# Pausing a fused attention and two-layer MoE kernel twice per block instead of four times

## What is computed

```python
# attention over chunks of 32 queries, 4 batches, 8 heads, 768 tokens, head size 64
k_full = concat(mem_k, k[l_start:r_end])          # 8 memory keys + up to 56 near keys
a = softmax(scale * q_c @ k_full.T);  out = a @ v_full
x = out as (3072, 512)
# first MLP
h = x @ w_in                                      # (3072, 2048)
g = h * sigmoid(h);  y = g @ w_out                # (3072, 512)
# soft MoE: 32 slots, 8 experts
logits = y @ phi                                  # (3072, 32)
d = softmax(logits, over tokens);  slot_input = d.T @ y
slot_out[e] = relu(slot_input[e] @ w1[e]) @ w2[e]
result = softmax(logits, over slots) @ slot_out
```

## Time and profile before

| | us |
|---|---|
| median of 3 executions | 465.17 (465.12 to 467.6) |
| profiled execution | 469.86 |
| span of the profiled execution | 467.9 |
| PE busy in that span | 448.6 |
| DVE busy | 276.7 |
| ACT busy | 138.9 |

### The profile page before, as it was taken

The page is one execution under the profiler, slowest core; times in us unless marked ns, Lnnn a source line. Parts: engine busy times, 40 slices in busy tenths (PEclk is TensorE's granted clock), DMA queues, the critical chain, the costliest instruction groups (busy, mean ns, idle before and its releaser), DMA issues.

```text
span 467.9 us, 12260 instructions
## 1 busy us (share of the span) xinstructions
PE 448.6 (96%) x5438; PEld 332.6 (71%) x5438; DVE 276.7 (59%) x540; ACT 138.9 (30%) x257; POOL 47.4 (10%) x44
## 2 busy tenths in 40 slices
PE   6799999999999999999999999999999999999990
PEld 5699777777876787767777777787677878543560
DVE  4567558765596566766665785568644557541142
ACT  2475233232331322332332323323222222210031
POOL 2576000000000000000000000000000000010000
PEclk9899999999999999999999999999999999999997
DMA  8996232321142143303321132130160479999997
GB/s 293 411 415 276 101 117 88 104 91 54 59 193 72 37 188 102 103 2 102 104 97 49 59 102 61 46 133 1 30 242 0 182 284 424 395 420 422 420 399 295
DMA packets 14820, 81.59 MB, mean 174 GB/s; under 512 B 1584, under 2 KB 1712, under 8 KB 8880
## 3 DMA queue, kind: packets, MB, share of 16 engines
q1 hardware_dynamic: 14768, 80.81, 45.0%
HBM read 74.51 MB, written 6.29 MB: 173 GB/s over the span
## 4 chain that ended last, share of the span: by engine, by line
PE 92%; DMA 3%; DVE 2%; issue 1%; ACT 0%; DVEq 0%
PE h_ps L310 57%; PE o_ps L294 5%; PE lpu_ps L327 5%; PE sx_ps L269 4%; PE lpu_ps L360 4%; DMA qk_sb<-qk 3%; PE sx_ps L360 2%; PE pt_ps L280 2%; PE sx_ps L699 2%; PE h_ps L1013 2%; PE lpu_ps L699 2%; PE h_ps L734 1%; PE h_ps L951 1%; PE o_ps L993 1%; PE lpu_ps L370 1%; PE pt_ps L1013 1%
## 5 line engine op out<-in xcount | busy, mean ns | idle before, releaser
L310 PE MATMUL h_ps<-x_odd,w_pair 128*128 128x512 f32 x576 | 138.3, 394 | 0.0
L310 PEld LDWEIGHTS h_ps<-x_odd,w_pair 128*128 128x128 f32 x576 | 106.3, 188 | 27.8 <-issue 4.6
L545 DVE SCALAR_TENSOR_TENSOR gT<-gT,h_ps 128x512 f32<-128x512 f32 (+1 forms) x108 | 66.1, 612 | 93.1 <-ACT gT L427 93.0
L427 ACT ACTIVATE gT<-h_ps 128x512 f32<-128x512 f32 (+1 forms) x108 | 58.4, 541 | 178.1 <-PE h_ps L310 177.4
L310 PE MATMUL h_ps<-x_even,w_pair 128*128 128x512 f32 x384 | 92.5, 395 | 0.0
L310 PEld LDWEIGHTS h_ps<-x_even,w_pair 128*128 128x128 f32 x384 | 70.9, 188 | 16.8 <-issue 1.7
L555 DVE STREAM_TRANSPOSE gB<-gT 128x512 f32<-128x512 f32 x80 | 56.7, 709 | 1.8
L310 PE MATMUL h_ps<-x_short,w_pair 128*128 128x256 f32 x384 | 51.6, 288 | 1.0 <-DVE gT L545 0.5
L310 PEld LDWEIGHTS h_ps<-x_short,w_pair 128*128 128x128 f32 x384 | 47.7, 192 | 6.0 <-issue 3.6
L529 POOL TENSOR_TENSOR sc<-sc,row_stats 128x512 f32<-128x512 f32 x23 | 24.0, 1044 | 275.0 <-DVE row_stats L523 275.0
L447 ACT ACTIVATE sc<-sc 128x512 f32<-128x512 f32 x23 | 14.6, 633 | 53.2 <-DVE sc L512 49.1
(11 more groups left out here) (193 smaller groups left out, 383.6 us busy)
## 6 DMA issues: line engine op xcount, KB each, us to landing
unit<-w SPq DMA_DIRECT2D x31, 1024.0 KB, 9.6
qk_sb<-qk SPq DMA_DIRECT2D x24, 640.0 KB, 5.4
v_sb<-v SPq DMA_DIRECT2D x24, 512.0 KB, 3.6
out<-unit SPq DMA_DIRECT2D x6, 1024.0 KB, 7.2
w_stage<-w_in SPq DMA_DIRECT2D x4, 1024.0 KB, 12.0
wot<-w_outT SPq DMA_DIRECT2D x4, 1024.0 KB, 12.7
unit<-w_out SPq DMA_DIRECT2D x4, 1024.0 KB, 5.3
unit_acc<-w SPq DMA_DIRECT2D x1, 1024.0 KB, 8.7
```

The costliest lines, as they stand in the source:

```text
L310: last = nc.tensor.matmul(h_ps[k % 2][:, 0:TOKS[b]], w_pair[:, k // 2, w, kc, k % 2 * 128:k % 2 * 128 + 128], x[:, lo, kc, 0:TOKS[b]], sta ...
L427: nc.scalar.activation(gt_of(b, k), h_ps[k % 2][:, 0:TOKS[b]], ACT.Tanh, scale=0.5).then_inc(tanh_done, 1)
L545: nc.vector.scalar_tensor_tensor(out=gt_of(b, k), in0=gt_of(b, k), scalar=1.0, in1=h_ps[k % 2][:, 0:TOKS[b]], op0=ALU.add, op1=ALU.mult).t ...
```

## The change

Long blocks pause twice, after chunks 1 and 9. A pause is values of two units, two logits steps (eight chunks of g) and scores of two units. The transposes of the pair stand apart: after chunks 7 and 8, and after chunk 15 and chunk 0 of the next block. The dispatch stays after chunk 4, now without transposes beside it. For this

- the ring of g has ten chunks; it takes the memory of the two early places, so no late weights are loaded in the middle any more. The list of places still has 23 entries of its own;
- scores of the two units of a pair lie beside each other in the same PSUM banks (`s_col`); DVE reads them only when both are written. Even units' values go to `o_ps`, odd units' to `pt_ps`; probabilities and `pt` have two buffers;
- block 0 keeps its pauses but scores units 3; 4; 5 and 6; 7 there, so that unit 6 follows unit 5 at once and units 6 and 7 are ready as a pair for block 1. Two logits steps follow its chunk 15 instead of three, behind the transposes of unit 6;
- SP loads both units' `qk` and then both units' `v`.

```diff
-GT_RING = 6
+GT_RING = 10
+LAST_RING = 12
+def pair_at(b, n):
+    if b >= LAST or 2 * n >= UNITS[b + 1]:
+        return ()
+    return (FIRST[b + 1] + 2 * n, FIRST[b + 1] + 2 * n + 1)
+def scored_at(b, n):
+    if b == 0:
+        return ((3,), (4,), (5, 6), (7,))[n]
+    return pair_at(b, 1) if n == 0 else pair_at(b + 1, 0)
...
+        def s_col(u):
+            return 4 * WIN * (u % 2) if u >= 2 else 0
...
         def pe_scores(pe, u, dispatched=0):
             pe.wait_ge(qk_in[u % QK_RING], 16 * (u // QK_RING + 1))
             if u >= 2:
-                pe.wait_ge(sc_done, u)
+                pe.wait_ge(sc_done, u - 1 if u >= PAIRED and u % 2 else u)
...
+        def pe_first_block(pe):
+            for k in range(NCH):
+                pe_mlp(pe, 0, k)
+                n = k // 4
+                if k % 4 == 1:
+                    pe_probs_T(pe, first_values(n))
+                if k % 4 == 2:
+                    for u in scored_at(0, n):
+                        pe_scores(pe, u)
+                    pe_values(pe, first_values(n))
+                if k == 11:
+                    pe_w2(pe)
+                if k == 12:
+                    pe_w2_T(pe)
+                if k == 15:
+                    pe_probs_T(pe, PAIRED)
+                    for m in range(2):
+                        pe_logits(pe, 0, m)
         def pe_block(pe, b):
             for k in range(NCH):
                 pe_mlp(pe, b, k)
...
+                n = k // 8
+                if k in (0, 8) and pair_at(b, n):
+                    pe_probs_T(pe, pair_at(b, n)[1])
+                if k == 2:
+                    pe_fold(pe, b - 1)
+                if k == DISPATCH_STEP:
+                    pe_dispatch(pe, b - 1, FIRST[b + 1] + 4 if b < LAST - 1 else NUN)
+                if k in (1, 9):
+                    for u in pair_at(b, n):
+                        pe_values(pe, u)
+                    if k == 1:
+                        pe_logits(pe, b - 1, 2)
+                        pe_logits(pe, b - 1, 3)
+                    elif b < LAST:
+                        pe_logits(pe, b, 0)
+                        pe_logits(pe, b, 1)
+                    for u in scored_at(b, n):
+                        pe_scores(pe, u, b if k > DISPATCH_STEP else 0)
+                if b == LAST and k in (5, 9, 13):
+                    pe_logits(pe, b, k // 4 - 1)
+                if k == 7 and pair_at(b, 1):
+                    pe_probs_T(pe, pair_at(b, 1)[0])
+                if k == 15 and pair_at(b + 1, 0):
+                    pe_probs_T(pe, pair_at(b + 1, 0)[0])
...
         def dve_scores(dve, u):
-            dve.wait_ge(s_mm, u + 1)
+            dve.wait_ge(s_mm, u + 2 if u >= PAIRED + 2 and u % 2 == 0 else u + 1)
...
-            nc.vector.memset(pt[:], 0.0).then_inc(pt_zero, 1)
+            nc.vector.memset(pt_all[:], 0.0).then_inc(pt_zero, 1)
...
-        EARLY = 2
-        places = [(13, p_tr, 2), (12, w2t_mm, 1), (6, h_mm, NCH * (LAST - 1))] + [(i, o_mm, NUN) for i in range(3)]
-        places += [(3, h_mm, NCH * LAST), (4, h_mm, NCH * LAST)]
-        for m in range(NCH // 2):
-            places.append((14 + m, h_mm, NCH * LAST + 2 * (m + 1)))
-            if m == 1:
-                places += [(i, u_mm, NB - 1) for i in (9, 10, 11)]
-        places += [(5, h_mm, NCH * NB), (7, u_mm, NB), (8, u_mm, NB), (22, uf_mm, 1)]
+        places = [(7, h_mm, NCH * (LAST - 1))] + [(i, o_mm, NUN) for i in range(4)]
+        places += [(4, h_mm, NCH * LAST), (5, h_mm, NCH * LAST), (13, h_mm, NCH * LAST + 2), (21, parthi_done, LAST)]
+        places += [(14, h_mm, NCH * LAST + 4)] + [(i, u_mm, NB - 1) for i in (10, 11, 12)]
+        places += [(13 + m, h_mm, NCH * LAST + 2 * (m + 1)) for m in range(2, NCH // 2)]
+        places += [(6, h_mm, NCH * NB), (8, u_mm, NB), (9, u_mm, NB), (22, uf_mm, 1)]
...
-            for u in range(7, NUN):
+            load_qk(7)
+            load_v(7)
+            for u in range(8, NUN, 2):
                 load_qk(u)
+                load_qk(u + 1)
                 load_v(u)
-                if u in (12, 14):
-                    load_unit((u - 12) // 2)
-            for u in range(EARLY, len(places)):
+                load_v(u + 1)
+            for u in range(len(places)):
                 load_unit(u)
```

More of the change, by code:

```diff
@@ L145, in moe_program @@
-        stage = at("w_stage", R + 14 * HALF_W, [128, NCH // 2, 2, KC, 256])
-        units = [at(f"unit{i}", R + i * HALF_W, [128, HALF_W]) for i in range(22)]
+        sc_all = at("sc", R, [128, SB, 2 * PAIRS, WIN])
+        pt_all = at("pt", R + 1024, [128, SB, 4 * PAIRS, QT])
+        qk_sb = at("qk_sb", R + 3072, [128, QK_RING, 2, QKW])
+        v_sb = at("v_sb", R + 3072 + QK_RING * 2 * QKW, [128, V_RING, 2, H * D])
+        assert 3072 + QK_RING * 2 * QKW + V_RING * 2 * H * D <= 4 * HALF_W
@@ L147, in moe_program @@
+        stage = at("w_stage", R + 13 * HALF_W, [128, NCH // 2, 2, KC, 256])
+        units = [at(f"unit{i}", R + i * HALF_W, [128, HALF_W]) for i in range(21)]
+        units.append(at("unit_gT", 4800 + 6 * TMAX, [128, HALF_W]))
         units.append(at("unit_acc", 1536, [128, HALF_W]))
-        fold_r = at("fold_r", R + 22 * HALF_W, [128, 128], fp32r)
-        w2_last = at("w2_last", R + 22 * HALF_W + 128, [128, 128])
+        wot = [units[i] for i in (10, 11, 12, 7)]
+        fold_r = at("fold_r", R + 21 * HALF_W, [128, 128], fp32r)
@@ L344, in pe_fold @@
             if b == LAST - 1:
[L345 removed]
+                pe.wait_ge(x_done, NUN)
             pe.wait_ge(fold_rounded, 1)
@@ L613, in dve_w2_T, with dve_first_block @@
             nc.vector.tensor_copy(w2c[:], heads(lp_ps[:])).then_inc(w2_done, 1)
+        def dve_first_block(dve):
+            for k in range(NCH):
+                n = k // 4
+                if k % 4 == 3:
+                    dve_sums(dve, scored_at(0, n)[0])
+                if k == 12:
+                    dve_sums(dve, PAIRED)
+                dve_g(dve, 0, k)
+                if k % 4 == 2:
+                    dve_scores(dve, scored_at(0, n)[0])
+                    dve_x(dve, first_values(n))
+                if k == 10:
+                    dve_scores(dve, PAIRED)
+                if k == 11:
+                    dve_w2(dve)
+                if k == 12:
+                    dve_w2_T(dve)
+                dve_gb(dve, 0, k)
         def dve_block(dve, b):
             for k in range(NCH):
-                n, at_pause = k // 4, k % 4 == pause(b)
-                if k % 4 == pause(b) + 1 and scores_at(b, n) is not None:
-                    dve_sums(dve, scores_at(b, n))
-                if b and k == 3:
+                n = k // 8
+                pair, scored = pair_at(b, n), scored_at(b, n)
+                if k in (2, 10) and scored:
+                    dve_scores(dve, scored[1])
+                if k == 3:
                     dve_et(dve, b - 1)
-                if 0 < b < LAST and k == 3:
+                if k == 3 and b < LAST:
                     dve_raw(dve, b - 1, range(4))
@@ L841, in _ @@
             act_wh(act, 2)
-            for b in range(NB):
+            act_first_block(act)
+            for b in range(1, NB):
                 act_block(act, b)
@@ L883, in _ @@
             dve_sums(dve, 2)
-            for b in range(NB):
+            dve_first_block(dve)
+            for b in range(1, NB):
                 dve_block(dve, b)
@@ L965, in _ @@
             keep_busy(4, h_ps[0])
-            for b in range(NB):
+            pe_first_block(pe)
+            for b in range(1, NB):
                 pe_block(pe, b)
```

182 lines of the change are left out of this document (87 added, 95 removed).

## The result

The changed kernel takes 470.25 us (median of 4, 468.57 to 473.37) against 465.7 for the kernel before: ratio 1.0102, 95% interval 1.0074 to 1.013. It is 1% slower, where 461.4 and faster was forecast.

A forecast was written before the change was run, and what follows sets the result against it. PE was taken to bound the middle and DMA the end. Gains of 1.40 + 1.44 + 0.64 + 2.20 - 0.20 = 5.5 us, less a 1.7 halt, took 465.17 to 461.4 us; range 459.5 to 464.8.

The forecast's parts named there:

- The middle's gain: From about 40 to 367 us, where PE never waits: merged pauses gain 5.5 us; a long block takes some 61.7.
- Logits joins: Long blocks' logits steps in pairs: each join saves 0.14 us, 10 pairs, 1.4 us.
- the values': Values of two units in a row: each join saves 0.16 us, 9 pairs, 1.44 us.
- the scores': Scores of two units in a row: each join saves 0.08 us, middle of 0 and 0.14; 8 pairs, 0.64 us.
- the edges against the MLP: Blocks 1 to 5, 20 pauses become 10: entering and leaving each costs the MLP 0.22 us, so 2.2 us gained.
- What costs nothing, and what hides it: Copies, ring, DVE work and loads around double pauses are hidden; slack 1.8 us for g, about 0.8 at the dispatch.
- Block 0: Unit 6's scores behind unit 5's wait for DVE and the qk load: PE halts once, 1.7 us lost.
- rival 1: After block 0's halt the clock drops, costing 1.7 us more: 463.1 us; chance 12%.
- The tail: DMA sets the end; two later megabytes fit the gap in blocks 5 and 6, so the gain comes through whole.
- Rival 5: DVE's two subtractions hold PE at 9 double pauses, likeliest at the dispatch: 12.6 us lost, 474 us; chance 7%.
- Rival 4: Overhead belongs to each matmul, so merging saves nothing and block 0's halt remains: 466.9 us; chance 5%.
- The excess of before's profiled execution: Whole profiled execution before the change: 4.7 us above the others' median, assumed to belong to profiling and to stay.

The follow-up runs named there:

- e9_best: Changed kernel with unit 6's scores after chunk 12 of block 0 and ten one-column products at the start: 460.71 us, ratio 0.9883 to the kernel before.
- e2_shift: Changed kernel with ten one-column products (40 PE instructions) put into the halt of block 0: 465.22 us, ratio 0.9972 to the kernel before.
- e4_split: Changed kernel with a pair's scores parted, one unit ahead of the values, the other behind the logits: 465.64 us, ratio 0.9982 to the kernel before.
- e7_fill: Changed kernel with ten full products of 128 columns (40 PE instructions) in the halt of block 0: 463.87 us, ratio 0.9954 to the kernel before.
- e8_before_shift: Control: the kernel before with ten one-column products behind unit 5's scores: 466.46 us against 466.0, ratio 1.0023.
- e1_apart: Changed kernel with unit 6's scores after chunk 12 of block 0, not right behind unit 5's: 465.77 us, ratio 0.9993 to the kernel before.
- e6_late_v: Changed kernel with unit 6's scores after chunk 12 and a pair's v loads issued only after its scores: 462.13 us, ratio 0.9909 to the kernel before.
- e5_period: Changed kernel with unit 6's scores after chunk 12 and 64 one-column products (256 instructions) in block 0: 472.35 us, ratio 1.0139 to the kernel before.

## Why the prediction was wrong

**The middle's gain** was right: a block takes 61.6 where 61.7 was forecast and 62.9 was measured before, in blocks 2, 3 and 4 alike. Logits joins measured 0.13 for 0.14, the values' 0.14 for 0.16, the scores' 0.14 for 0.08: the upper bound, not the middle. Those three make 0.41 of the 0.65 that a pause saves; the other 0.24 is what the edges against the MLP and the dispatch give together, for 0.22 less 0.02. 5.5 was summed and 5.5 is also what e9_best keeps, but with 0.7 of products in it, so this match is partly luck.

**The step that failed** is "What costs nothing, and what hides it". It asked ACT, DVE, the ring and the data loads for slack, and costed the supply of PE's own instructions at nothing without naming it. It measured 4.2 us: four of the eight pauses with double scores. It needed two things that both were in the change: twice the scores in a row, and two v loads issued together 2.7 us ahead of them, whose data flow while the code packet should come. The single pauses of before had 128 score instructions and one v load, whose data begin with the scores and not before them, and no such wait in their trace, so the trace of before showed no cost; it did show the packets and their number.

**Block 0** was right in its mechanism and wrong in size. "Loss: 1.7 us" was the halt; it measured 2.4 in the profiled execution and up to 4.1 in another run. DVE's part came out at 1.7 as summed. The load is what was mis-sized: its landing was taken from one execution as if fixed, 8.9 us, and measured 9.8. And rival 1, the clock that drops after the halt, was given 12%; it is what happened. The reason given, that one halt between full work is too little idle, was an argument without a row: the only drop at hand had more idle ahead of it, which says nothing of less.

Together: -5.5 + 2.4 + 1.5 + 4.2 = +2.6, which from 465.7 gives 468.3; the profiled execution took 468.57. The median is 1.7 above that. Longer halts can account for it: from the end of unit 5's scores to the start of unit 6's it is 2.4 us here, and 3.4, 4.1 and 4.0 in e2_shift, e4_split and e7_fill, which have the same halt. But the unprofiled executions don't show their waits, and the last block and tail, 100.6 us here, lie between 99.1 and 101.4 in the profiled executions of all kernels. So this part stays open.

**The tail** was right: it takes the two later megabytes into its gap. From the dispatch after chunk 4 in the last block to the end of the span it is 90.5 us in the changed kernel (376.1 to 466.6) and 90.9 before. Rival 5 didn't come: no wait for g or for the kept logits after a double pause (the 0.5 us for g in the list of waits stands in before's too). Rival 4, overhead of each matmul, falls with the joins.

**The excess of before's profiled execution**, 4.7 us, was assumed to belong to profiling. It was mostly the wait and the clock at the start, about 3.8 together by those rows: block 1 began at 61.16 there and at 58.59 in e8_before_shift, which has 0.7 of products ahead of it and no such wait. Of the other profiled executions e1_apart's alone had such a drop of the clock.

## What to carry to other kernels

Before putting short matmuls together, count PE's instructions per microsecond in the densest stretch: here 256 in 1.4 us used up the code before the next packet was there, with data loads in the way. Where a late "issue" wait shows in the middle of a run of equal matmuls, look at when the code packet starts against the data loads; shift the code by some tens of instructions, and by 256 as a check; then move the loads out of the way or part the dense groups. A shift alone is fragile, since any later edit moves the borders again. A halt of PE has a price besides its length, the clock after it, and a profiled execution before a change should be searched for such accidents before its total is used.

## What the runs showed of the hardware

- The kernel changes of speed with the place of its code. Forty instructions that compute nothing made the changed kernel 5 us faster (470.25 to 465.22), of which 4.2 are the four waits. The halts lie a whole number of 256 instructions apart. The Trainium skill, page "Runtime: NRT & Kernel Launch", section Instruction fetch mechanics, says that code comes in blocks of 256 instructions and that the cost of crossing one is mostly hidden; the number of packets agrees (43 for some 11,000), the hiding held in the kernel before and failed here by up to 1.4 us at a time (e1_apart).
- The code packets come by the DMA engines that carry the data, and late behind it: behind two v loads the packet started 1.4 us later against the scores than with free engines (e6_late_v), and ahead of the loads' data 2.3 us before the scores (e2_shift). From its start to PE going on it took 2.4 us.
- The clock fell to its lower level after a halt of 2.4 us, and stayed up where 2.5 us of full products left a halt of 1.5. It also fell behind 128 matmuls of one column, with PE listed as busy throughout (0.50 over four microseconds, e5_period): being listed as busy did not keep it up.
